# The last expert's gate logits summed ahead of its rows, and the wait for the result's last rows moved from GpSimd to VectorE

## The chip, the cores and the metric

One core of one Trainium2 chip runs the whole program. The metric is the device time of one execution in microseconds (us). Engine names as in the rows: PE is TensorE's matrix multiply, PEld its weight loads (the two overlap), DVE is VectorE, ACT is ScalarE, POOL is GpSimd, SP is the sync engine; a "q" behind a name (POOLq, SPq) is the engine's own queue of waits, branches and DMA issues.

## The reference, cut to what matters

Attention over 2 batches of 768 tokens comes first; its result, 1536 rows of 512 numbers, goes through two mixture-of-experts layers with 8 experts each. The first layer (`_moe_ref`) gives every expert exactly 192 tokens. The second one takes the first one's rows:

```
skip_score = x @ w_skip                 # rows with skip_score <= 0 pass unchanged
logits = x @ w_gate                     # 1536 x 8
e_idx  = argmax(logits); gate = softmax(logits)[e_idx]
out[i] = x[i] + gate * (relu(x[i] @ w1[e_idx]) @ w2[e_idx])
```

So nothing of the second layer can be placed before the first layer's rows have been multiplied with `w_gate` (8 columns) and `w_skip` (1 column). The kernel keeps the nine columns together.

## The kernel before, in words

`middle` is the first expert layer. Its work is a list of steps written out by `middle_plan`, and every engine walks the same list in that order and takes from it what is its own. For an expert k the steps are `xt` (transpose the gathered tokens), `h` (first matmuls, line 1006), `y` (second matmuls, line 1020, into transposed rows yT of 4 blocks d = 0 to 3, copied to SBUF by ACT at line 1093 two blocks at a time) and `rw` (line 1035). An `rw` step multiplies 96 rows of yT, two blocks of them, with `pw2`, 137 columns wide: 128 are an identity and turn the rows round, 9 are the gate columns. There are four `rw` steps per expert (two halves i of 96 rows, two pairs a of blocks). ACT copies from each first the partial logits into `lg4` (line 1100) and then the rows into `x1` (line 1101). For expert 7 nothing is left to fill the time, so its `rw` steps stand alone at the end of the list. All float32 matmuls appear as two records each in the trace: 8 matmuls of line 1035 are "x16".

`regroup` places rows for the second layer, in three batches; the third is the two row blocks of expert 7 (`place`, NI - 2, 2). DVE (`vector`) sums the four partial logits (line 1350), takes the best expert (lines 720 to 724), makes the one-hot O2 (line 1357), waits until PE has counted (`tensor`: four small bf16 matmuls, lines 1433 to 1439), computes places (lines 1362 to 1366) and a selection matrix `sel` (line 1370), and then the records (up to line 1384), which POOL scatters to DRAM (line 1455, two DMAs). `totals` (line 1446) is one bf16 matmul with 8 columns, which DVE's `table` waits for: the table says which further tiles run and is read by the engines late in the second layer.

`experts2` is the second layer. Its tile 0 is mixed: most rows come early by a gather (line 1546), transposed by `first_rows` (line 1552) into a PSUM bank, and expert 7's rows are added to the same bank by `last_rows` (line 1561) with `sel`. ACT copies the bank out (line 1692), then `hidden` (line 1650) and `rows` (line 1664) follow for every tile. Tiles from 1 on are gathered by POOL (line 1578) once SP has loaded their records (line 1615); `transposes` (line 1637) runs on PE between the two parts of `rows`. DVE adds (line 1709) into `ob`, POOL scatters `ob` to the output (line 1586). `tiles` is the helper that unrolls these steps for an engine, with a branch for the tiles that may not exist; its argument `last` is called after everything else of the tile, and it is `landed` for POOL: a wait until the scatter's data have landed. `K["warm"](bank, n)` issues n bf16 matmuls of 512 columns whose result nobody reads. They stand after `first_rows` (5) and at the head of `last_rows` (6). Before `last_rows`, PE waits for `sel` and for the last `x1` copy.

At the program's end (the block that ends at line 1723 in the trace) every engine runs a DRAIN, then all meet at a semaphore.

Of the kernel before, what the change touches and what calls it, by code (L numbers as in the profile page):

```python
# [10 lines left out]
ALU = mybir.AluOpType  # L11
ACT = mybir.ActivationFunctionType
AX = mybir.AxisListType
# [3 lines left out]
N, DM, E, F = B * S, H * D, 8, 1024  # L17
# [11 lines left out]
KD, KF = DM // P, F // P  # L29
# [575 lines left out]
HT = CAP // 2  # L605
# [19 lines left out]
def middle_plan():  # L625
# [67 lines left out]
    for k in range(ROUNDS - 1, E):  # L693
# [6 lines left out]
        steps += todo  # L700
    steps += [("rw", E - 1, i, a) for i in range(2) for a in range(2)] + [("place", NI - 2, 2)]
    return steps
# [24 lines left out]
def middle(nc, io, sb, sem, K, link):  # L727
# [73 lines left out]
    s_w1, s_w2 = K["s_w1"], K["s_w2"]  # L801
    K["s_lg"] = sem("logits_copied")
    K.update(s_x1=s_x1, s_x1l=s_x1l, s_f=s_f, s_e=s_e, s_tok=s_tok, use=use)
# [96 lines left out]
    def tensor(pe, place):  # L900
        for st in steps:
# [109 lines left out]
            elif st[0] == "y":  # L1011
# [11 lines left out]
                if part and d % 2:  # L1023
                    ins.then_inc(s_f, 1)
            elif st[0] == "rw":

                _, k, i, a = st
                ps = enter(pe, use[st])
                if i == 0 and a == 0:
                    pe.wait_ge(s_e, emptied(("y", k, KD // 2 - 1)))  # L1030
                    if k == 0:
                        pe.wait_ge(K["s_const2"], K["n_const2"])
                for c in range(2):
                    d = 2 * a + c
                    ins = nc.tensor.matmul(ps[0:HT, c * 137:c * 137 + 137], yT[:, k % 2, d, i * HT:(i + 1) * HT],  # L1035
                                           K["pw2"][:, d, :], start=True, stop=True)
                ins.then_inc(s_f, 1)
            elif st[0] == "place":
                place(pe, *st[1:])


    def scalar(act, place):
        for st in steps:
# [51 lines left out]
            elif st[0] == "rw":  # L1095
                _, k, i, a = st
                n = use[st]
                act.wait_ge(s_f, n + 1)
                v = psW[n % NWB][0:HT, 0:274].rearrange("p (c t) -> p c t", c=2)
                nc.scalar.copy(lg4[:, 2 * k + i, 2 * a:2 * a + 2, :], v[:, :, 128:137]).then_inc(K["s_lg"], 1)  # L1100
                nc.scalar.copy(x1[:, 2 * k + i, 256 * a:256 * a + 256].rearrange("p (c t) -> p c t", c=2),
                               v[:, :, 0:128]).then_inc(s_e, 1)
            elif st[0] == "place":
                place(act, *st[1:])
# [190 lines left out]
def regroup(nc, io, sb, sem, K, link):  # L1295
# [46 lines left out]
    def vector(dve, i0, n):  # L1342
# [3 lines left out]
        if b == 0:  # L1346
            nc.vector.memset(cum[:, :], 0.0)
            link(dve, nc.vector.memset(cumb[:, :], 0.0))
        dve.wait_ge(K["s_lg"], 2 * (i0 + n))
        link(dve, nc.vector.tensor_reduce(lg[:, 0:n, :], lg4[:, i2, :, :].rearrange("p i k n -> p i n k"), AX.X, ALU.add))  # L1350
        l8 = lg[:, 0:n, 0:E]
# [71 lines left out]
    def tensor(pe, i0, n):  # L1423
        if i0 + n == NI:
            K["first_rows"](pe)
            K["warm"](K["psA"][1][:, 0, :], 5)
        pe.wait_ge(s_o2, batches[i0, n] + 1)
# [10 lines left out]
        for k in range(1, n):  # L1438
            ins = nc.tensor.matmul(psP[0:HT, k * E:n * E], K["onesb"][0:HT, 0:HT], Of[:, 0:(n - k) * E], start=False,
                                   stop=k == n - 1, skip_group_check=True)  # L1440
        ins.then_inc(s_pp, 1)

    def totals(pe):
# [24 lines left out]
def experts2(nc, io, sb, sem, K):  # L1468
# [86 lines left out]
    def last_rows(pe):  # L1555
        K["warm"](K["psA"][1][:, 0, :], 6)
        pe.wait_ge(K["s_sel"], 1)
# [9 lines left out]
    def pool(gp):  # L1567
# [21 lines left out]

        def landed(t):  # L1590
            gp.wait_ge(s_st[t % 2], 16 * (t // 2 + 1))

        tiles(gp, gather, store, landed, ahead=2)

# [32 lines left out]
    def tensor(pe):  # L1627
        def transposes(t):
            if t == 0:
                last_rows(pe)  # L1630
                K["totals"](pe)
                return
# [49 lines left out]
        for t in range(E - 1):  # L1682
            hidden(t)
            rows(t, 0, 6)
            transposes(t + 1)
            rows(t, 6, KF)
# [15 lines left out]
    def vector(dve):  # L1702
# [9 lines left out]

        tiles(dve, nothing, add)

# [232 lines left out]
```

## Time and profile before

| | |
|---|---|
| time, median of 3 runs | 669.04 us (668.77 to 669.31) |
| the profiled execution's own time | 669.03 us |
| its span, first to last instruction | 667.2 us |
| PE busy | 637.5 us, 96% |
| PEld busy | 500.7 us, 75% |
| DVE, ACT, POOL busy | 366.5, 293.6, 155.8 us |
| mean granted TensorE clock | 0.994 of full |
| chain that ended last | PE 85%, issue 4%, DVE 4%, ACT 2% |

The profiled execution lies 1.8 us above its span and agrees with the median. PE is busy in nearly all of the span, so a change counts where PE waits: at the join of the layers (about 517 to 526 us), and after PE's last matmul (656.4 us), where the span goes on for 10.8 us. A timeline row gives start, length, engine, line, what is done, and in brackets how long the engine had been idle and what released it.

### The profile page before, as it was taken

The page shows a single profiled execution, that of the slowest core. Times are in us where ns is not written, and L with a number is a line of the kernel's source. Part 1 is how long each engine was busy: PE and PEld are TensorE (multiplying, and loading weights), DVE is VectorE, ACT ScalarE, POOL GpSimd, SP SyncE. Part 2 cuts the span into 40 slices and gives each one's busy share as a digit, 9 for nine tenths or more (in the row PEclk, how much of TensorE's full clock was granted, in tenths as well). Part 3 has the DMA queues.
Part 4 walks back from the last instruction along what each step waited for, and adds up shares of the span by engine and source line. Part 5 has one row for each costly group of instructions (what it writes and reads, how often), then busy time and mean ns, then how long its engine had stood idle before and what let it go on. Part 6 is the DMA issues. An engine that isn't in the chain of part 4 may idle for free.

```text
span 667.2 us, 11738 instructions
## 1 busy us (share of the span) xinstructions
PE 637.5 (96%) x4544; PEld 500.7 (75%) x4544; DVE 366.5 (55%) x1114; ACT 293.6 (44%) x551; POOL 155.8 (23%) x151
## 2 busy tenths in 40 slices
PE   6899999999999999989999999999999999999993
PEld 3667777777777665468898988989999766777771
DVE  5876777676776677787787868585301400000000
ACT  4767676767677667143543525251321211111110
POOL 5440313031320943201010101101161232223100
PEclk9999999999999999999999999999999999999997
DMA  8975646454562300554362717354996599999910
GB/s 205 227 170 127 145 99 160 121 119 119 121 197 63 77 21 1 201 171 151 128 201 77 273 57 246 133 169 151 342 331 225 171 312 357 362 335 325 330 69 8
DMA packets 73758, 118.40 MB, mean 177 GB/s; under 512 B 33400, under 2 KB 36600, under 8 KB 73426
## 3 DMA queue, kind: packets, MB, share of 16 engines
q1 hardware_dynamic: 69298, 108.65, 52.6%
q0 software_dynamic: 4080, 8.93, 4.0%
q8 instruction: 38, 0.62, 0.4%
q14 instruction: 22, 0.18, 0.1%
q10 hardware_dynamic: 320, 0.01, 0.0%
HBM read 88.07 MB, written 12.36 MB: 151 GB/s over the span
## 4 chain that ended last, share of the span: by engine, by line
PE 85%; issue 4%; DVE 4%; ACT 2%; POOL 1%; DMA 1%; SPq 0%; DVEq 0%; POOLq 0%
PE psB L1006 13%; PE psB L1020 12%; PE psB L1650 10%; PE psB L1664 9%; PE psB L311 8%; PE psB L296 8%; PE psA L281 6%; PE psA L283 4%; PE psB L1035 2%; PE psA L940 2%; PE psB L326 2%; PE psB L258 2%; PE psB L250 1%; DVE mx L431 1%; PE psB L1793 1%
## 5 line engine op out<-in xcount | busy, mean ns | idle before, releaser
L431 DVE TENSOR_REDUCE mx<-psA 128x1 f32<-128x768 f32 x96 | 91.8, 957 | 48.7 <-PE psA L283 47.1
L549 ACT ACTIVATE prob<-psA,ebi,esc 128x768 f32<-128x768 f32 x96 | 95.8, 998 | 30.6 <-DVE ebi L377 30.6
L1006 PE MATMUL psB<-xgT,w 128*128 128x192 f32 x512 | 92.8, 332 | 3.0 <-ACT xgT L1080 3.0
L1006 PEld LDWEIGHTS psB<-xgT,w 128*128 128x128 f32 x512 | 82.4, 190 | 9.0 <-ACT xgT L1080 3.7
L1020 PE MATMUL psB<-hT,w 128*128 128x192 f32 x512 | 88.6, 329 | 0.0
L1020 PEld LDWEIGHTS psB<-hT,w 128*128 128x128 f32 x512 | 82.7, 190 | 0.3
L296 PE MATMUL psB<-cst,prob 128*128 128x128 f32 x576 | 78.8, 273 | 0.4
L281 PE MATMUL psA<-kH,qT 128*128 128x384 f32 x192 | 74.1, 386 | 1.9 <-DMA kB<-kbits 1.1
L542 ACT COPY pT<-psB 128x512 f32<-128x512 f32 x96 | 56.5, 588 | 41.1 <-PE psB L296 39.9
L1709 DVE SCALAR_TENSOR_TENSOR ob<-psB,recs,xg 128x512 f32<-128x512 f32 x9 | 6.8, 751 | 121.1 <-PE psB L1664 121.1
L296 PEld LDWEIGHTS psB<-cst,prob 128*128 128x128 f32 x576 | 67.6, 140 | 6.4 <-DVE pT L444 2.3
L1650 PEld LDWEIGHTS psB<-xgT,w 128*128 128x128 f32 x576 | 65.6, 192 | 4.7 <-issue 4.7
L311 PE MATMUL psB<-pT,v_in 128*64 128x384 f32 x360 | 68.0, 499 | 0.0
L1650 PE MATMUL psB<-xgT,w 128*128 128x128 f32 x576 | 65.8, 275 | 0.8 <-ACT xgT L1692 0.8
L283 PE MATMUL psA<-kB,qB 128*128 128x384 f32 x192 | 64.9, 338 | 0.0
L1664 PE MATMUL psB<-w,hT 128*128 128x512 f32 x144 | 64.6, 592 | 0.0
L281 PEld LDWEIGHTS psA<-kH,qT 128*128 128x128 f32 x192 | 36.1, 188 | 30.7 <-issue 28.1
L1250 POOL DMA_INDIRECT xg<-x_scratch,sidx x16 | 15.3, 958 | 182.5 <-DVE sidx L1142 180.0
L1664 PEld LDWEIGHTS psB<-w,hT 128*128 128x128 f32 x144 | 26.0, 190 | 26.3 <-issue 26.3
L571 POOL CAST hi<-raw 128x768 fp32r<-128x768 f32 x16 | 14.1, 890 | 127.2 <-ACT raw L522 111.0
L1086 ACT ACTIVATE hT<-psB 128x384 f32<-128x384 f32 x32 | 15.7, 491 | 60.4 <-PE psB L1006 60.2
L1697 ACT ACTIVATE hT<-psB 128x512 f32<-128x512 f32 x18 | 10.8, 597 | 68.4 <-PE psB L1650 68.4
(259 smaller groups left out, 903.5 us busy)
## 6 DMA issues: line engine op xcount, KB each, us to landing
w<-in_moe_w SPq DMA_DIRECT2D x34, 2048.0 KB, 9.6
kH<-hi SPq DMA_DIRECT2D x30, 192.0 KB, 3.5
q_in<-in_q SPq DMA_DIRECT2D x16, 192.0 KB, 3.5
k_in<-in_k SPq DMA_DIRECT2D x16, 192.0 KB, 4.0
v_in<-in_v SPq DMA_DIRECT2D x8, 384.0 KB, 3.4
x_scratch<-x_of_batch SPq DMA_DIRECT2D x2, 1536.0 KB, 6.9
x_scratch<-x SPq DMA_DIRECT2D x8, 384.0 KB, 10.6
qT<-hi SPq DMA_DIRECT2D x15, 192.0 KB, 3.5
```

The lines of the kernel that those rows point to most:

```text
L281: nc.tensor.matmul(psS[u % 2][:, half, 0:HALF], qT[:, i, hh, qs], kH[:, i, hh, ks], start=True, stop=False)
L283: ins = nc.tensor.matmul(psS[u % 2][:, half, 0:HALF], qB[:, i, hh, qs], kB[:, i, hh, ks], start=False, stop=True)
L296: ins = nc.tensor.transpose(psT[part][:, at * P:(at + 1) * P], prob[:, u % 2, c // GU, c % GU * P:(c % GU + 1) * P], cst[:, C_ID:C_ID + P])
L311: ins = nc.tensor.matmul(psV[64 * hh:64 * hh + 64, 0:HALF], v_in[:, i, hh, c, :], pT[:, (2 * G + hh) % 4, c, :], start=c == 0, stop=c == N ...
L431: nc.vector.tensor_reduce(mx[:, u:u + 1], psS[u % 2][:, :, 0:HALF], AX.XY, ALU.max).then_inc(s_dv, 1)
L542: nc.scalar.copy(pT[:, (2 * G + hh) % 4, TD:NC_, c * P:(c + 1) * P], psT[1][:, 0:(NC_ - TD) * P].rearrange("p (c q) -> p c q", c=NC_ - TD) ...
L549: ins = nc.scalar.activation(prob[:, u % 2, :, :], psS[u % 2][:, :, 0:HALF], ACT.Exp, bias=ebi[:, u:u + 1], scale=esc[:, u:u + 1], accum_o ...
L1006: ins = nc.tensor.matmul(ps[:, (f % 2) * CAP:(f % 2 + 1) * CAP], w1[:, k % 2, d, f * P:(f + 1) * P], xgT[:, k % 2, d, :], start=d == 0, st ...
L1020: ins = nc.tensor.matmul(ps[:, (d % 2) * CAP:(d % 2 + 1) * CAP], w2[:, k % 2, f, d * P:(d + 1) * P], hT[:, k % 2, f, :], start=f == 0, sto ...
L1086: nc.scalar.activation(hT[:, k % 2, f - 1:f + 1, :], psW[n % NWB][:, 0:2 * CAP].rearrange("p (c t) -> p c t", c=2), ACT.Relu).then_inc(s_e, 1)
L1650: ins = nc.tensor.matmul(psH[q][:, f * P:(f + 1) * P], w1[:, k2 % 2, k, (4 * q + f) * P:(4 * q + f + 1) * P], xT[:, t % 2, k, :], start=k ...
L1664: ins = nc.tensor.matmul(psY[t % 2][:, :], hh[:, t % 2, f, :], w2[:, k2 % 2, f, :], start=f == 0, stop=f == KF - 1)
```

## The change

In the plan, a step `logits` stands before expert 7's `rw` steps. It sums expert 7's gate and skip logits in PSUM, 4 blocks by 2 halves, 8 float32 matmuls with 9 moving columns; blocks 0 and 1 only need the first yT copy. DVE waits for that (semaphore `s_ll`) and takes the sum from PSUM with one copy in place of the reduction; ACT no longer copies the partial logits of expert 7. `first_rows` moves behind the counting matmuls; both `warm` calls (11 matmuls) go; `totals` moves from behind `last_rows` to behind `hidden(0)`. In `experts2`, `landed` moves from POOL to DVE.

```diff
-    steps += [("rw", E - 1, i, a) for i in range(2) for a in range(2)] + [("place", NI - 2, 2)]
+    steps += [("logits", )] + [("rw", E - 1, i, a) for i in range(2) for a in range(2)] + [("place", NI - 2, 2)]
...
+    K["psLog"] = psRow[1][0:HT, 0:2 * NW]
...
+            elif st[0] == "logits":
+                k = E - 1
+                for d in range(KD):
+                    if d % 2 == 0:
+                        pe.wait_ge(s_e, emptied(("y", k, d // 2)))
+                    for i in range(2):
+                        ins = nc.tensor.matmul(K["psLog"][:, i * NW:(i + 1) * NW], yT[:, k % 2, d, i * HT:(i + 1) * HT],
+                                               K["pw2"][:, d, 128:128 + NW], start=d == 0 and i == 0,
+                                               stop=d == KD - 1, skip_group_check=True)
+                ins.then_inc(K["s_ll"], 1)
...
-                nc.scalar.copy(lg4[:, 2 * k + i, 2 * a:2 * a + 2, :], v[:, :, 128:137]).then_inc(K["s_lg"], 1)
+                if k < E - 1:
+                    nc.scalar.copy(lg4[:, 2 * k + i, 2 * a:2 * a + 2, :], v[:, :, 128:137]).then_inc(K["s_lg"], 1)
...
-        dve.wait_ge(K["s_lg"], 2 * (i0 + n))
-        link(dve, nc.vector.tensor_reduce(lg[:, 0:n, :], lg4[:, i2, :, :].rearrange("p i k n -> p i n k"), AX.X, ALU.add))
+        if i0 + n < NI:
...
+        else:
+            dve.wait_ge(K["s_ll"], 1)
+            link(dve, nc.vector.tensor_copy(lg[:, 0:n, :], K["psLog"].rearrange("p (i n) -> p i n", n=NW)))
...
     def tensor(pe, i0, n):
-        if i0 + n == NI:
-            K["first_rows"](pe)
-            K["warm"](K["psA"][1][:, 0, :], 5)
         pe.wait_ge(s_o2, batches[i0, n] + 1)
...
         ins.then_inc(s_pp, 1)
+        if i0 + n == NI:
+            K["first_rows"](pe)
...
     def last_rows(pe):
-        K["warm"](K["psA"][1][:, 0, :], 6)
         pe.wait_ge(K["s_sel"], 1)
...
-        def landed(t):
-            gp.wait_ge(s_st[t % 2], 16 * (t // 2 + 1))
-
-        tiles(gp, gather, store, landed, ahead=2)
+        tiles(gp, gather, store, ahead=2)
...
                 last_rows(pe)
-                K["totals"](pe)
                 return
...
             hidden(t)
+            if t == 0:
+                K["totals"](pe)
             rows(t, 0, 6)
...
-        tiles(dve, nothing, add)
+        def landed(t):
+
+            dve.wait_ge(s_st[t % 2], 16 * (t // 2 + 1))
+
+        tiles(dve, nothing, add, landed)
```

## Rows read from the trace of the kernel before

**Rows 1.** The page, part 4: chain that ended last, by engine.
```profile
PE 85%; issue 4%; DVE 4%; ACT 2%; POOL 1%; DMA 1%; SPq 0%; DVEq 0%; POOLq 0%
```

**Rows 2.** Timeline of the join: start, length, engine, line, [idle before <-releaser].
```profile
506.35 10.56 PE L1020 MATMUL psB<-hT,w 128*128 128x192 f32 x64
...
517.54 1.89 PEld L1035 LDWEIGHTS psB<-pw,yT 128*96 128x96 f32 x16 [0.93 <-ACT yT L1093]
517.57 2.09 PE L1035 MATMUL psB<-pw,yT 128*96 128x137 f32 x16 [0.66 <-ACT yT L1093]
...
519.61 0.97 PEld L1552 LDWEIGHTS psA<-cst,xg 128*128 128x128 f32 x8 [0.18 <-DMA xg<-x_scratch,recs]
...
519.77 0.37 ACT L1101 COPY x<-psB 96x256 f32<-96x256 f32 x1
...
520.28 0.17 DVE L720 TENSOR_REDUCE best<-lg 96x2 f32<-96x16 f32 x1
...
521.80 0.12 PEld L1433 LDWEIGHTS psA<-O,strictb 96*96 96x96 bf16 x1 [0.45 <-DVE O L1357]
...
522.25 0.17 DVE L1362 TENSOR_TENSOR tmp<-psA,cst 96x16 f32<-96x16 f32 x1 [0.43 <-PE psA L1439]
...
523.59 1.86 PEld L1561 LDWEIGHTS psA<-sel,x 96*128 96x128 f32 x16 [0.62 <-DVE sel L1370]
...
525.67 0.59 ACT L1692 COPY xgT<-psA 128x512 f32<-128x512 f32 x1 [3.96 <-PE psA L1561]
...
526.40 7.38 PE L1650 MATMUL psB<-xgT,w 128*128 128x128 f32 x64 [0.76 <-ACT xgT L1692]
```

**Rows 3.** Instruction groups, 517.4 to 526.4 us: count | busy us, mean ns.
```profile
L1793 PE MATMUL psA<-onesb 128*128 128x512 bf16 x11 | 2.7, 378 | 0.0
```

**Rows 4.** The timeline at 492 us: a run of float32 weight loads.
```profile
492.38 0.80 PEld L992 LDWEIGHTS psB<-cst,xg 96*128 96x128 f32 x8
```

**Rows 5.** Timeline, 520 to 539 us: what feeds the second tile.
```profile
520.22 0.33 SPq L1264 DMA_DIRECT2D x_scratch<-x  x1
...
526.52 0.92 POOL L1455 DMA_INDIRECT records<-rec,posi  x1 [0.30 <-issue]
...
529.07 2.25 SPq L1615 DMA_DIRECT2D recs<-records  x5
...
533.20 0.96 POOL L1578 DMA_INDIRECT xg<-x_scratch,recs  x1 [0.30 <-issue]
...
533.82 0.38 SPq L1596 DMA_DIRECT2D w<-in_moe_w  x1
...
538.84 0.42 PEld L1637 LDWEIGHTS psA<-cst,xg 128*128 128x128 f32 x4 [0.72 <-DMA xg<-x_scratch,recs]
```

**Rows 6.** DMA issues, 517-532 and 476-495 us: last number is landing.
```profile
x_scratch<-x SPq DMA_DIRECT2D x1, 384.0 KB, 8.4
...
records<-rec,posi POOLq DMA_INDIRECT x2, 2.8
...
records<-rec,posi POOLq DMA_INDIRECT x10, 7.4
```

**Rows 7.** Busy time by stretch, with PEclk, DMA share, GB/s last.
```profile
526.00:527.00 1.00, 0.59 (x5) 0.63 (x6) 0.90 (x4) 0.26 (x1) 0.69 (x2) 1.00 0.36 130
...
659.00:660.00 1.00, 0.00 (x0) 0.00 (x0) 0.00 (x0) 0.00 (x0) 0.00 (x0) 0.67 0.24 84
```

**Rows 8.** Lines L1723 and L1510: count: duration ns min/median/max, first and last start.
```profile
L1723 DVEq DRAIN  x1: 582/582/582, 656.7 to 656.7; - x1
...
L1723 POOLq DRAIN  x1: 5547/5547/5547, 661.5 to 661.5; - x1
...
L1510 POOLq COMPARE_BRANCH  x1: 38/38/38, 660.6 to 660.6; - x1
```

**Rows 9.** The timeline at the end: the last two operations.
```profile
656.43 0.75 DVE L1709 SCALAR_TENSOR_TENSOR ob<-psB,recs,xg 128x512 f32<-128x512 f32 x1 [13.26 <-PE psB L1664]
657.98 0.98 POOL L1586 DMA_INDIRECT out<-ob,recs  x1 [13.00 <-DVE ob L1709]
```

More of the change, by code:

```diff
@@ L801, in middle @@
     s_w1, s_w2 = K["s_w1"], K["s_w2"]
-    K["s_lg"] = sem("logits_copied")
+    K["s_lg"], K["s_ll"] = sem("logits_copied"), sem("last_logits")
+    K["psLog"] = psRow[1][0:HT, 0:2 * NW]
     K.update(s_x1=s_x1, s_x1l=s_x1l, s_f=s_f, s_e=s_e, s_tok=s_tok, use=use)
@@ L1348, in vector @@
             link(dve, nc.vector.memset(cumb[:, :], 0.0))
-        dve.wait_ge(K["s_lg"], 2 * (i0 + n))
-        link(dve, nc.vector.tensor_reduce(lg[:, 0:n, :], lg4[:, i2, :, :].rearrange("p i k n -> p i n k"), AX.X, ALU.add))
+        if i0 + n < NI:
+            dve.wait_ge(K["s_lg"], 2 * (i0 + n))
+            link(dve, nc.vector.tensor_reduce(lg[:, 0:n, :], lg4[:, i2, :, :].rearrange("p i k n -> p i n k"), AX.X,
+                                              ALU.add))
+        else:
+            dve.wait_ge(K["s_ll"], 1)
+            link(dve, nc.vector.tensor_copy(lg[:, 0:n, :], K["psLog"].rearrange("p (i n) -> p i n", n=NW)))
         l8 = lg[:, 0:n, 0:E]
```

## The prediction

> **What bounds the kernel now.** I read the chain that ended last first: 85% of it is PE and the rest is waits of a few tenths [rows 1]. So an edit pays only where PE stands still with nothing queued, or behind its last matmul. Then the timeline of the join. Expert 7's last `y` matmul ends at 506.35 + 10.56 = 516.91. ACT copies it, and PE's `rw` steps start at 517.57 (0.66 idle) and end at 519.66 [rows 2]. After that PE has `first_rows` (from 519.61) and 11 matmuls that only fill time [rows 2, 3]; what the next layer really waits for is a chain that crosses engines: `rw` full, ACT copies the last logits, DVE reduces them and begins its choice at 520.28, PE counts at 521.80, DVE goes on at 522.25, `sel` lets `last_rows` start at 523.59, ACT copies at 525.67, `hidden` starts at 526.40 [rows 2]. From there on PE is fed without a break but for one short wait (0.72 on the weight-load side at 538.84, for the second tile's gather [rows 5]). So every tenth by which that chain starts earlier is a tenth of the time, until another input is late. Last the tail: DVE's last add ends at 656.43 + 0.75 = 657.18, POOL issues the last scatter at 657.98 to 658.96 [rows 9], its queue wakes on the landing at 660.6, begins its DRAIN at 661.5 and needs 5.547 us for it; all else is long done [rows 8]. That ends the span at 667.2.
>
> **The join, step by step.** The new `logits` step has 8 matmuls, 16 records, with yT as weights (128x96, as in `rw`) and only 9 moving columns, so weight loads set its pace. No row has such a matmul. The dearest near row is `rw` itself with 137 columns: 1.89 / 16 = 0.118 us a record [rows 2]. A run with 96 moving columns goes at 0.80 / 8 = 0.10 [rows 4]. The lower end is that it costs nothing, since half of it fits into the 0.66 us that PE idles anyway. I take 0.10, the nearest in columns and in what limits it: from 516.91, 8 records to 517.71 (the gap is gone), 8 more to 518.51; the yT copy is in by 517.54, so the second half doesn't wait.
>
> The `rw` steps then end at 518.51 + 2.09 = 520.60, 0.95 later than before. DVE starts its copy when the last logits matmul is through, about 0.3 after its load (518.8), and this costs about what a 96x16 read of PSUM costs, 0.17 [rows 2], so the choice begins at about 519.0 and not at 520.28: 1.28 earlier. Counting could then start at 521.80 - 1.28 = 520.52, and PE's queue is free at 520.60. The two meet; I book 521.80 - 520.60 = 1.2. At 0.118 a record PE is the later one: 516.91 + 1.89 + 2.09 = 520.89, which leaves 0.9. At a price of zero PE is free at 519.66 and the gain is at most 2.1. Both ends go into the range.
>
> The Trainium skill (TensorE: Matmul & The Clock Gate, section LDWEIGHTS) says a weight load takes its columns divided by 1.2, in ns, whatever the rows, so 80 ns for 96 columns. By that the step would take 16 x 0.08 = 1.28 us and the join would gain 1.5 instead of 1.2. No row here shows a load at that pace, the nearest goes at 0.10, so the sum doesn't use it.
>
> Behind the count nothing is longer than it was. `first_rows` (a run that begins at 519.61 and takes about 1.1 with the matmuls' tail) now stands between count and `last_rows`: it runs from about 520.8 to 521.9, inside the time in which DVE makes `sel` (before: 521.80 to 523.59, 1.79 [rows 2]; now 520.6 to 522.4). That cover is 0.5 longer than it needs. Its gather had landed at 519.6 [rows 2], over a microsecond before it is now wanted; if the cover were gone it would cost up to 1.1. The two `warm` runs, 2.7 busy us in all [rows 3], stood wholly in waits, so taking them out gives and costs nothing in itself. ACT's last row copy (519.77 before [rows 2]) comes at about 520.7 and ends at 521.1, ahead of `last_rows` at 522.4. ACT has four small copies less, which nobody waited for any more. `totals` stood in a wait of PE; now it stands between two full runs: one more bf16 load, as the 0.12 of line 1433 [rows 2], so minus 0.1. DVE's table starts some 7 us later than now and nobody reads it before the second half of the layer, and DVE's next add comes at about 540; so nothing.
>
> What is late next is the second tile. The chain of records moves with DVE: second scatter at 526.52 - 1.2 = 525.3, records loaded from 529.07 - 1.2, gather from 533.20 - 1.2 [rows 5]. The weights of line 1596 (533.82) move as well, as they wait for PE, so the two compete as before [rows 5]. But two things don't move: the DMA engines are full until 526 to 527 [rows 7], so the scatters are now in that crowd, and the last `x1` store goes from 520.22 to about 521.1 and lands 8.4 later [rows 5, 6], at 529.5 at most (before: 528.6). POOL waits for it ahead of its gathers; it would look at it from 529.8. That holds by 0.3. A few tenths of delay to the gather, 0 to 0.5, are likely and partly already in the 0.72; I take 0.1. The join is then worth 1.2 - 0.1 - 0.1 = 1.0, from 0.4 to 1.9.
>
> **The tail.** POOL now has no wait for landings. Its engine is free at 658.96 [rows 9]. Whether its queue gets to the DRAIN at once or after its branches isn't shown; they and the waits took 661.5 - 660.6 = 0.9 before [rows 8]. DVE's DRAIN starts at 656.7, inside its last add that ends at 657.18, so a queue does run ahead of its engine [rows 8, 9]. Whatever DRAIN does for 5.547 us, POOL had been idle for 2.5 us when it began [rows 8, 9]: it didn't wait for POOL's own instruction. If the length is its own, it now ends between 658.96 + 5.55 = 664.5 and 0.9 later, where it was 667.0: a gain of 1.6 to 2.5, and I take 2.2. DVE takes the wait over: behind it there is only its DRAIN. Landing at 660.6 plus 0.9 for the same waits plus 0.58 is 662.1, over 2 us ahead of POOL, so that costs nothing; if POOL's DRAIN were short, DVE would end the span.
>
> A sentence on what could be inside: the Trainium skill (GPSIMD Engine Reference, section Instruction dispatch) says that the first call of a freshly loaded routine pays about 6 us with no instruction to be seen; that would make the length fixed, and the sum the same. No row here shows that a load takes place.
>
> **Sum.** 669.03 (the profiled execution, 667.2 span and 1.8 around it; the median is 669.04) - 1.0 - 2.2 = 665.8.
>
> **The rivals.**
> (a) As above: 665.8, by itself 664.8 to 667.0. Chance 0.55.
> (b) The DRAIN only begins its 5.55 us when the last data have landed: 660.6 + 5.55 = 666.15 and not 667.0, 0.9 gained, 667.1 in all. For it: all that is outstanding then is that scatter. Against it: before, nothing was outstanding, and it was long even so. Chance 0.15.
> (c) The edit of the tail does nothing: the end of the DRAIN hangs on the last DMA instruction (8.0 us after its end now), not on when the DRAIN starts. Then only the join counts: 669.03 - 1.0 = 668.0. For it: 5.5 us on an idle engine look like waiting for something. Chance 0.20.
> (d) Slower: the scatters of records, now issued at 524.1 and 525.3 into full DMA engines, land 7.4 us after issue, as in the crowd at 476 to 495 us, and not 2.8 [rows 6]. Records, gather and the second tile's transposes would be 4.6 later, and PE would stand at about 537.5 for that long: 669.03 - 1.0 + 4.6 - 2.2 = 670.4. It decides once the crowd lasts to 529 us or so. Against it: at 526 to 527 the engines are busy for only 0.36 [rows 7], and the bytes are the same. Chance 0.05.
> (e) Slower or no gain: without the fill matmuls the clock falls at the join. After the last matmul at 656.4 the granted clock is at its full level (2.4 GHz) still for over two microseconds and falls to the half in 659 to 660 [rows 7]. PE's longest rests at the join would be about 0.5 to 0.8, as now, and at 526 to 527, after such a rest, the clock was full [rows 2, 7]. If it fell, `hidden(0)`'s 7.38 us would take up to as much again, 670 and more. The rule of the Trainium skill (TensorE: Matmul & The Clock Gate, Part 1) that activity holds the clock up speaks against taking filler out; the rests are too short here for me to give it more than this. Chance 0.05.
>
> **How the numbers follow.** The forecast is (a), 665.8. The range must leave out no more than 2 in 10: from 664.7 (the join at 1.8, the tail at 2.5) to 668.3 (case (c) with a weaker join); (d), (e) and the edges lie outside. What a measurement of this kernel can tell from no change is 0.2%, 1.3 us, so below 667.7 is faster: (a), nearly all of (b) and a third of (c), 0.76. Same: the rest of (c) and some of (b) and (e), 0.16. Slower: 0.08.
>
> **What the profile after should show.** Line 1350's reduction is gone for this batch and DVE's choice begins near 519.0. The logits run lasts about 1.6 with no idle time ahead of it; if it lasts 1.9, the join gives 0.9. `last_rows` starts near 522.4, `hidden` near 525.2. At line 1637's first run, the wait for the gather is at most 1.2; if it is several us, (d). Granted clock 1.00 from 518 to 530; if not, (e). POOL's DRAIN begins at 659 to 660 and lasts 5.5: (a). If it lasts 7: (b). If it ends 8 us after the scatter's end whatever its start: (c). The forecast is wrong by most if the DRAIN's length isn't its own.

## The result and the profile after

| | before | changed |
|---|---|---|
| median of 5 runs | 669.04 us | 666.74 us |
| lowest to highest | 668.77 to 669.91 | 664.87 to 670.08 |
| ratio | | 0.9963, 95% interval 0.9945 to 0.9982 |
| profiled execution, span and own time | 667.2, 669.03 | 668.3, 670.08 |

The changed kernel is 2.3 us faster in the median. Its five executions spread over 5 us and those of the kernel before over 1, and the profiled execution is its slowest. Some executions of several kernels ran far slower (745, 925, 2251 us); medians and ratios here leave them out.

With more executions the difference in spread is smaller: 24 of the kernel before lie within 3.5 us (668.2 to 671.6, standard deviation 1.0), 12 of the changed one within 5.8 (e10_after below, 1.7). Part of the spread comes from ahead of the join. There, in this profile, the granted clock was at half (1.2 GHz) for 3.4 us from 288.3 on, and the first 16 matmuls of line 1009 took 4.52 us (first row); in e3_hold (described below), with the clock full, they took 2.84 (second row):

```profile
287.56 4.52 PE L1009 MATMUL psB<-xgT,w 128*128 128x192 f32 x16 [0.33 <-ACT xgT L1093]
```

```profile
288.16 2.84 PE L1009 MATMUL psB<-xgT,w 128*128 128x192 f32 x16 [0.33 <-ACT xgT L1093]
```

So the profile is read against the end of the last `y` matmul: 507.41 + 10.56 = 517.97, before 516.91 [rows 2], 1.06 later. But for the first weight loads of the logits nothing of the change stands ahead of that mark, and it lies between 516.9 and 519.4 from one kernel's profile to the next on the chips of the first result and of the first and last experiments.

The timeline of the changed kernel at the join and through its second tile:

```profile
507.41 10.56 PE L1023 MATMUL psB<-hT,w 128*128 128x192 f32 x64
...
517.65 1.65 PEld L1034 LDWEIGHTS psA<-pw,yT 128*96 128x96 f32 x16
...
518.01 0.48 ACT L1106 COPY yT<-psB 128x384 f32<-128x384 f32 x1 [4.72 <-PE psB L1023]
...
519.24 2.10 PE L1048 MATMUL psB<-pw,yT 128*96 128x137 f32 x16
...
519.70 0.17 DVE L721 TENSOR_REDUCE best<-lg 96x2 f32<-96x16 f32 x1
...
521.22 0.12 PEld L1449 LDWEIGHTS psA<-O,strictb 96*96 96x96 bf16 x1
...
521.42 1.14 PE L1570 MATMUL psA<-cst,xg 128*128 128x128 f32 x8
...
523.00 2.05 PE L1578 MATMUL psA<-sel,x 96*128 96x128 f32 x16 [0.44 <-DVE sel L1389]
...
525.82 7.38 PE L1663 MATMUL psB<-xgT,w 128*128 128x128 f32 x64 [0.77 <-ACT xgT L1707]
525.93 0.92 POOL L1473 DMA_INDIRECT records<-rec,posi  x1 [0.30 <-issue]
529.67 2.24 SPq L1629 DMA_DIRECT2D recs<-records  x5
...
533.23 0.38 SPq L1610 DMA_DIRECT2D w<-in_moe_w  x1
...
533.49 0.96 POOL L1595 DMA_INDIRECT xg<-x_scratch,recs  x1 [0.30 <-issue]
...
540.67 0.93 PE L1650 MATMUL psA<-cst,xg 128*128 128x128 f32 x4 [2.21 <-DMA xg<-x_scratch,recs]
...
541.39 3.35 PE L1677 MATMUL psB<-w,hT 128*128 128x512 f32 x4
```

The sum of logits (line 1034) begins ahead of the last `y` matmul's end. The rows' `rw` steps (line 1048) start 1.27 after it, DVE's choice (line 721) at +1.73 (519.70; before 520.28 - 516.91 = +3.37), the count (line 1449) at +3.25 (before +4.89), `last_rows` (line 1578) at +5.03 (before +6.68), `hidden` (line 1663) at 525.82 - 517.97 = +7.85, before +9.49 [rows 2]. So TensorE is 1.64 us ahead as it enters the second layer. Then it loses all of it and more: the second tile's transposes (line 1650) wait 2.21 us for their gather, and the matmuls behind them take 3.35 for 4 where four like them take 1.88 elsewhere. The stretches of the same execution (PE, PEld, DVE, ACT, POOL busy, then PEclk, DMA share, GB/s) show why:

```profile
539.00:540.60 1.60, 0.00 (x0) 0.00 (x0) 0.00 (x0) 0.00 (x0) 0.00 (x0) 1.00 1.03 422
540.60:542.00 1.40, 1.32 (x5) 1.06 (x6) 0.00 (x0) 0.36 (x1) 0.00 (x0) 0.61 0.77 313
542.00:544.00 2.00, 2.00 (x4) 0.72 (x3) 0.00 (x0) 0.22 (x1) 0.00 (x0) 0.50 0.00 0
544.00:545.00 1.00, 1.00 (x6) 0.71 (x5) 0.22 (x1) 0.00 (x0) 0.00 (x0) 0.83 0.00 0
545.00:546.00 1.00, 1.00 (x11) 1.00 (x10) 0.53 (x1) 0.00 (x0) 0.00 (x0) 1.00 0.07 20
```

TensorE stood still from about 538.5 to 540.7. A mean of 0.61 over the 1.4 us from 540.6 is full clock (2.4 GHz) for 0.3 and half (1.2 GHz) for the rest, so it fell at 540.9; by the 0.83 it came back at about 544.3. The DMA engines are full (share 1.03) while TensorE waits for the gather; in this execution the wait was followed by a second loss, through the clock.

The tail, the last two operations and the DRAINs (kind, count, duration ns, start):

```profile
659.96 0.75 DVE L1724 SCALAR_TENSOR_TENSOR ob<-psB,recs,xg 128x512 f32<-128x512 f32 x1 [13.26 <-PE psB L1677]
661.50 0.98 POOL L1603 DMA_INDIRECT out<-ob,recs  x1 [13.00 <-DVE ob L1724]
```

```profile
L1742 POOLq EVENT_SEMAPHORE  x2: 17/17/17, 668.1 to 668.2; - x2
...
L1742 POOLq DRAIN  x1: 6603/6603/6603, 661.4 to 661.4; - x1
...
L1742 DVEq DRAIN  x1: 17/17/17, 665.0 to 665.0; - x1
```

POOL's DRAIN starts at 661.4, ahead of the scatter it stands behind, and ends at 668.0, 5.56 after the scatter's end at 662.48. Before, it ended 8.05 after it (661.46 + 5.55 against 658.96 [rows 8, 9]). VectorE is through at 665.0, 3 us earlier. The tail gives 2.5 us.

The three parts add up to the profiled execution. VectorE's last add starts 659.96 - 517.97 = 141.99 after the mark, before 656.43 - 516.91 = 139.52: 669.03 + 1.06 (ahead of the join) + 2.47 (join to last add) - 2.49 (tail) = 670.07, measured 670.08.

### The profile page after: what moved, and what is told of

Its sections match the earlier page's. It is cut to its first block, busy times and chain, and to the rows that moved or that the text cites. A ratio compares the mean times of both kernels' runs of the same rounds, so it can differ in the third digit from the quotient of the medians.

```text
span 668.3 us, 11743 instructions
## 1 busy us (share of the span) xinstructions
PE 638.6 (96%) x4549; PEld 503.6 (75%) x4549; DVE 366.5 (55%) x1114; ACT 292.9 (44%) x547; POOL 155.1 (23%) x151
## 4 chain that ended last, share of the span: by engine, by line
PE 80%; DMA 5%; issue 4%; DVE 4%; SPq 3%; ACT 2%; POOL 2%; POOLq 0%; DVEq 0%
PE psB L1009 14%; PE psB L1023 12%; PE psB L1677 9%; PE psB L1663 9%; PE psB L311 8%; PE psB L296 7%; PE psA L281 5%; PE psA L283 4%; PE psB L1048 2%; PE psA L943 2%; PE psB L326 2%; DMA xg<-x_scratch,recs 1%; DMA kB<-kbits 1%; PE psB L1812 1%; PE psB L250 1%
## 5 line engine op out<-in xcount | busy, mean ns | idle before, releaser
L1009 PE MATMUL psB<-xgT,w 128*128 128x192 f32 x512 | 94.5, 336 | 3.0 <-ACT xgT L1093 3.0
L1009 PEld LDWEIGHTS psB<-xgT,w 128*128 128x128 f32 x512 | 84.1, 193 | 9.0 <-ACT xgT L1093 3.7
L1663 PEld LDWEIGHTS psB<-xgT,w 128*128 128x128 f32 x576 | 65.8, 192 | 5.1 <-issue 5.1
L1677 PE MATMUL psB<-w,hT 128*128 128x512 f32 x144 | 66.2, 604 | 0.0
```

The costliest lines, as they stand in the source:

```text
L1009: ins = nc.tensor.matmul(ps[:, (f % 2) * CAP:(f % 2 + 1) * CAP], w1[:, k % 2, d, f * P:(f + 1) * P], xgT[:, k % 2, d, :], start=d == 0, st ...
L1663: ins = nc.tensor.matmul(psH[q][:, f * P:(f + 1) * P], w1[:, k2 % 2, k, (4 * q + f) * P:(4 * q + f + 1) * P], xT[:, t % 2, k, :], start=k ...
L1677: ins = nc.tensor.matmul(psY[t % 2][:, :], hh[:, t % 2, f, :], w2[:, k2 % 2, f, :], start=f == 0, stop=f == KF - 1)
```

## The experiments

**The two edits apart.** e1_tail is the kernel before with this alone:

```diff
-        def landed(t):
-            gp.wait_ge(s_st[t % 2], 16 * (t // 2 + 1))
-        tiles(gp, gather, store, landed, ahead=2)
+        tiles(gp, gather, store, ahead=2)
...
-        tiles(dve, nothing, add)
+        def landed(t):
+            dve.wait_ge(s_st[t % 2], 16 * (t // 2 + 1))
+        tiles(dve, nothing, add, landed)
```

> The kernel before with one edit: VectorE and not GpSimd waits for the result's rows (the function landed). In the changed kernel GpSimd's DRAIN began at 661.4, inside the last scatter (661.50 to 662.48), and ended 5.56 us after the scatter's end; before it ended 8.05 us after it. Theory A (DRAIN costs its own 5.55 us as soon as the engine is free): 2.5 us faster than before, 666.5, with as little spread as before (about 1 us). Theory B (part of what the changed kernel won at the tail was something of that one execution): less than 1 us faster, DRAIN ends 8 us after the scatter.

Measured: 666.57 us median, the kernel before beside it 669.28; ratio 0.9960 (0.9945 to 0.9975), so 1.7 to 3.7 us faster. Its executions spread over 4.1 us (665.5 to 669.61), without any of the join's edits. The last scatter and the DRAIN:

```profile
658.18 0.98 POOL L1586 DMA_INDIRECT out<-ob,recs  x1 [13.00 <-DVE ob L1706]
```

```profile
L1724 POOLq DRAIN  x1: 6603/6603/6603, 658.1 to 658.1; - x1
```

The DRAIN ends 5.56 after the scatter, as in the changed kernel. The tail's edit is worth 2.5 us in both profiles, and the median agrees.

e2_join is the changed kernel with that edit taken back (the diff above the other way round).

> The changed kernel with GpSimd waiting for landings again, so only the join's edits are left. Theory A (the race: TensorE reaches the second tile's transposes 1.6 us earlier, the gather for them comes only 0.8 earlier and now starts behind the 2 MB weight load that TensorE's progress releases; by execution it lands in time or up to 3 us late, and after a long wait the clock falls as well): between 667.4 (in time) and 672.6, a spread of some 5 us, median about 669.2, no faster than before. Theory C (the spread comes from the head of the program, the half-clock stretch at 288 us, and the join's gain is whole): 1.6 us faster, 667.4, with a second cluster 1 us above.

Measured: 669.66 against 669.28, ratio 1.0002 (0.9986 to 1.0019). Ten of its runs lie between 667.3 and 671.5, one at 673.0. So the join's edits give nothing that the median can show, though they make `hidden` start 1.64 earlier in each profile of theirs. My second theory, that the spread comes from the half-clock stretch near 288 us and the join's gain is whole, holds only in its first half: the stretch is in this profile too (289.3 to 292.7), but a whole gain would have shown in the median. The profile has the mild form of the late gather, a wait of 0.51 us at line 1653:

```profile
530.38 2.25 SPq L1632 DMA_DIRECT2D recs<-records  x5
...
534.20 0.96 POOL L1595 DMA_INDIRECT xg<-x_scratch,recs  x1 [0.30 <-issue]
...
534.62 0.38 SPq L1613 DMA_DIRECT2D w<-in_moe_w  x1
...
540.36 0.66 PE L1653 MATMUL psA<-cst,xg 128*128 128x128 f32 x4 [0.51 <-DMA xg<-x_scratch,recs]
```

**The late gather.** In e3_hold SyncE waits for it before it issues the weights that compete with it:

```diff
                 sp.wait_ge(s_h, 2 * (t - 1))
+                if t == 2:
+                    sp.wait_ge(s_g[1], 16)
                 w1_load(sp, t, io["moe2_w1"][bass.ds(e, 1), :, :])
```

> The changed kernel; SyncE waits until the second tile's rows have been gathered before it issues the third tile's first weights (line 1610, t = 2). Theory A (the race with the weight load): the gather lands about 3 us earlier than in the changed kernel's profile (537.5 and not 540.6), TensorE's wait at line 1650 is under 0.3 us, no half-clock stretch at 541; 664.9, all executions within 1 us but for the head's stretch at 288 us (+1). Theory C (the gather is late because its records are late, not because of the weights): the wait stays over 1 us and the spread stays. The weights themselves are wanted 18 us later, so holding them for 3 us costs nothing in either.

Measured: 664.9 (663.96 to 666.07) against 669.28, ratio 0.9925 (0.9906 to 0.9945). The gather is issued at 532.18, the weights at 535.82, the transposes (line 1652) start at 537.19 with no wait, the clock is full there:

```profile
528.34 3.10 SPq L1629 DMA_DIRECT2D recs<-records  x5
...
532.18 0.96 POOL L1595 DMA_INDIRECT xg<-x_scratch,recs  x1 [0.30 <-issue]
...
535.82 0.38 SPq L1610 DMA_DIRECT2D w<-in_moe_w  x1
...
537.19 0.60 PE L1652 MATMUL psA<-cst,xg 128*128 128x128 f32 x4
```

That is 1.7 us below e1_tail and 1.8 below the changed kernel: with the gather in time the join's gain is whole. The transposes start 20.34 after the last `y` matmul's end (516.85); in the changed kernel's profile 540.67 - 517.97 = 22.70.

e4_swap goes at it from the other side. The second tile's records and gather go first and nothing waits:

```diff
         def gather(t):
+            t = 1 - t if t < 2 else t
             gp.wait_ge(s_rl[t], 16)
...
                 sp.wait_ge(K["s_rsl"], 16 * 2)
+            t = 1 - t if t < 2 else t
```

> The changed kernel; GpSimd gathers the second tile's rows before those that VectorE adds to the first tile, and SyncE loads the second tile's records first. Nothing waits for the weights. Theory A (the second tile's gather comes too late behind the weight load): it is issued 1.3 us earlier, at about the same distance ahead of the weights as in the kernel before, TensorE's wait at line 1650 is 0 to 0.5 us, PE ends 137.8 to 138.4 us after the last y matmul (changed kernel's profile: 141.95), median 664.9 to 665.5. Theory C (the wait is set by the records alone): the gather moves by 1.3 all the same, so this can't tell the two apart, but if the wait stays over 1 us in the profile neither holds.

This kernel, e6_drain, e7_tail_hold and e8_crowd ran on another chip, on which everything was some 9 us longer (the kernel before: 678.63), nearly all of it ahead of the join; only ratios compare. Measured: 0.9926 (0.9900 to 0.9952), as e3_hold; the gather is issued at 540.85, the weights at 541.68, and the transposes start at +20.35, no wait.

e7_tail_hold adds the hold of e3_hold to e1_tail.

> The kernel e1_tail (the kernel before with only the tail's edit) with the hold of e3_hold: the third tile's first weights wait for the second tile's gather. Theory A: in the kernel before the gather comes in time, so the hold brings 0 to 0.2 us: 666.6, PE ends 139.4 us after the last y matmul; the difference to e3_hold, 1.6 to 1.7 us, is then the join's gain when nothing takes it back. Rival: the hold itself is a gain of 1 us or more (weights that load in the gather's way also slow other things), 665.5 or less, and the join's edits are worth under 1 us even at their best.

Measured: 0.9951 (0.9932 to 0.9970); e1_tail had 0.9960. The difference, 0.6 us, is smaller than either interval, and the profiles show none: VectorE's last add starts 666.12 - 526.72 = 139.40 after the last `y` matmul, in e1_tail 656.64 - 517.23 = 139.41. So the hold alone brings nothing that shows. Beside it on the same chip e4_swap is at 0.9926, 0.0025 x 678.6 = 1.7 us better. The intervals overlap, but its profile has 137.89, 1.5 earlier, as have all six profiles with the join's edits and the gather in time (e3_hold, e4_swap, e6_drain, e8_crowd, e9_drain_early, e12_best: 137.9). That is the join with nothing taken back.

e10_after is the changed kernel again.

> The changed kernel once more, unchanged, beside the kernel before on the same chip, for another profile of the race. In the profiles so far the second tile's gather lands 7.1 us after its issue where the weights were issued 0.3 us ahead of it, 6.1 where they came 0.4 behind it, 5.6 at 0.6, 4.6 at 0.8 and 3.6 at 1.6 or held back. Theory A: this profile's gather lies on that line as well, and TensorE's wait follows from it; the executions spread over some 3 to 5 us, median 2.3 to 3 us below the kernel before, above e3_hold's 5. Rival (the first result was drawn down by single bad executions): median 4 us or more below the kernel before, as the kernels with the gather in time.

Measured: 667.07 against 669.0, ratio 0.9968 (0.9951 to 0.9984), 12 runs from 664.94 to 670.7. It is as in the first result, and the rival, that single bad executions had drawn the first result down, is out. The profile has a 3.26 us wait, on line 1650:

```profile
532.19 0.96 POOL L1595 DMA_INDIRECT xg<-x_scratch,recs  x1 [0.30 <-issue]
532.24 0.38 SPq L1610 DMA_DIRECT2D w<-in_moe_w  x1
...
540.73 0.66 PE L1650 MATMUL psA<-cst,xg 128*128 128x128 f32 x4 [3.26 <-DMA xg<-x_scratch,recs]
...
541.23 1.88 PE L1677 MATMUL psB<-w,hT 128*128 128x512 f32 x4
```

The weights were issued 0.05 us behind the gather, which landed 8.5 us after its issue. Here the clock stayed full, and the four matmuls took 1.88. The profiles side by side (gather and weights from the timelines; landing from the DMA view, where the trace has it; wait of TensorE's matmuls at the transposes):

| kernel | weights issued after the gather by | gather lands after | TensorE waits |
|---|---|---|---|
| changed | -0.26 | 7.1 | 2.21, and half clock |
| changed, again (e10_after) | 0.05 | 8.5 | 3.26 |
| e2_join | 0.42 | 6.1 | 0.51 |
| before | 0.62 | 5.6 | 0.1 (0.72 of the weight loads) |
| e11_before_drain | 0.66 | 5.8 | 0.2 |
| e1_tail | 0.81 | 4.6 | 0 |
| e4_swap | 0.83 | not in the trace | 0 |
| e5_warm | 1.61 | 3.6 | 0 |
| e9_drain_early, e12_best (held) | 3.4 | 3.3, 3.4 | 0 |
| e3_hold | 3.64 | 3.6 | 0 |

It isn't a line, as my expectation had it. With 0.8 us of lead or more the gather lands within 4.6 us, with less than 0.7 it takes 5.6 or more; among the late ones the order isn't strict, since the worst (8.5) had the weights just behind it and not ahead. And TensorE asks for the rows at +20.3 with the join's edits, at +21.9 without them, so the kernel before could bear 5.6 and the changed one can't. Each kernel has one profile, so how its other executions divide between the gather, the clock and the part ahead of the join isn't shown.

**What makes the gather lose its lead.** TensorE, and with it the weights, came 1.64 earlier; the gather only 0.77 (533.49 - 517.97 = +15.52, before 533.20 - 516.91 = +16.29) or 1.07 (e10_after, +15.22). The last scatter of records is a full 1.65 earlier (525.93: +7.96; before +9.61), but SyncE can load records only at +11.70, before +12.16: the scatter takes 3.74 to be seen and not 2.55 (in e10_after 3.43, in e2_join 3.06). In e8_crowd the 2 MB load that fills the DMA engines at that time comes later:

```diff
         sp.wait_ge(K["s_f"], K["use"][("y", E - 2 + t, KD // 2 - 1)] + 1)
-        w2_load(sp, t, io["moe2_w2"][t:t + 1])
+        if t == 0:
+            w2_load(sp, t, io["moe2_w2"][t:t + 1])
...
         def body(t):
+            if t == 1:
+                sp.wait_ge(s_g[1], 16)
+                w2_load(sp, t, io["moe2_w2"][t:t + 1])
```

> The changed kernel, but the second tile's second weights (2 MB, issued at 516.9 to 518.0 so far and filling the DMA engines until 526 to 527) are loaded only after the second tile's gather has landed. Theory F (that load is the crowd which holds up the scatters of the last records): the records land 2.5 us or less after the second scatter's start, as in the kernel before, and not 3.5 to 3.7; records are loaded by SyncE 1.0 us earlier against the last y matmul than in e3_hold (+10.5 and not +11.5), the gather as well; time 664.9 as e3_hold, since there TensorE doesn't wait any more. Rival (the landing is late for the scatter's own reasons): records load stays at +11.5.

```profile
534.00 0.92 POOL L1473 DMA_INDIRECT records<-rec,posi  x1 [0.30 <-issue]
536.80 1.77 SPq L1630 DMA_DIRECT2D recs<-records  x4
```

536.80 - 534.00 = 2.8, against 3.5 in e3_hold (528.34 against 524.82) and 3.74 in the changed kernel. Against the last `y` matmul (526.03) the records are loaded at +10.77 and not +11.49. In the nine profiles with the join's edits and that load in place the time is 3.06 to 3.91, so the load is most of the delay, 0.7 of it against e3_hold. Ratio 0.9925 (0.9900 to 0.9951), as e3_hold, since TensorE no longer waited there.

**The fill matmuls.** e5_warm puts them back where they stood:

```diff
             K["first_rows"](pe)
+            K["warm"](K["psA"][1][:, 0, :], 5)
...
     def last_rows(pe):
+        K["warm"](K["psA"][1][:, 0, :], 6)
```

> The changed kernel with its 11 fill matmuls put back, 5 behind first_rows and 6 ahead of last_rows. Theory A (they only stood in waits, and the late gather makes the slow executions): same median and same spread as the changed kernel, 665 to 670. Theory B (taking them out made the clock fall, and this is what costs): the spread goes, all executions near 664.9 to 665.5. A third possibility, that they now stand in the way since first_rows and they fill more than the wait for sel: 0.3 to 0.8 us slower than the changed kernel.

Measured: 666.9 (665.52 to 668.41), ratio 0.9956 (0.9937 to 0.9976). Of my three, the third possibility: the fill matmuls now stand in the way, and by more than I had put it. In the median it is no slower than the changed kernel, because that one loses as much to its late gather. The rows:

```profile
520.01 2.10 PE L1048 MATMUL psB<-pw,yT 128*96 128x137 f32 x16
...
525.55 1.95 PE L1580 MATMUL psA<-sel,x 96*128 96x128 f32 x16
```

`last_rows` (line 1580) starts 525.55 - 518.74 = +6.81 and not +5.03. Behind the count and `first_rows` the 11 matmuls run for 2.5 us, past the moment at which `sel` is ready, and take the join's whole gain back. The gather is in time for the same reason, so the kernel is e1_tail again in its times. It says nothing of the clock; there the profiles do: in none of e3_hold, e4_swap, e8_crowd, without fill matmuls, does the granted clock fall at the join (it is 1.00 from the last `y` matmul to the second tile).

**What a DRAIN costs.** e6_drain is e3_hold with one more, in the middle of the second layer:

```diff
                                   ).then_inc(s_st[t % 2], 16)
+            if t == 5:
+                gp.drain()
```

> The kernel e3_hold with one more DRAIN on GpSimd behind the sixth tile's scatter, in the middle of the second layer, where GpSimd has 8 us and more of rest. Theory D (a DRAIN behind a scatter takes 5.55 us each time): the extra one takes 5.5 to 6.6 us, hidden, the last one as well, time as e3_hold, 664.9. Theory E (only the first one of the program is dear, a routine that has to be brought in): the extra one 5.5 to 6.6 us, the last one under 1.5 us (its overlap with the scatter), 659.5 to 660.5, and VectorE's wait for the landing ends the span instead.

```profile
L1607 POOLq DRAIN  x1: 9182/9182/9182, 624.8 to 624.8; - x1
```

```profile
L1746 POOLq DRAIN  x1: 2911/2911/2911, 667.8 to 667.8; - x1
...
L1746 DVEq DRAIN  x1: 17/17/17, 671.4 to 671.4; - x1
```

The extra one takes 9.2 us in a rest of GpSimd, where both theories had 5.5 to 6.6; the last one takes 2.9 and ends 1.9 behind the scatter's end, which fits neither. VectorE's starts at 671.4 and ends the span. Ratio 0.9890 (0.9865 to 0.9914). Whether the first DRAIN is dear, or each one in proportion, was for e9_drain_early (the extra DRAIN behind the first layer's gathers):

> The kernel e3_hold with the extra DRAIN on GpSimd not in the second layer but behind the last of the 16 gathers of the first one, ahead of 51 of the 67 DMAs that GpSimd issues. In e6_drain (7 DMAs between the two DRAINs) the last DRAIN ended 1.9 us after the last scatter's issue and not 5.6. Theory E (a routine is brought in once, and was lost after the DRAIN at the program's start): the last one is as short as in e6_drain, 1.9 us after the scatter, VectorE ends the span, 2.5 to 3 us faster than e3_hold. Theory G (a DRAIN works off what the DMAs since the DRAIN before have left behind): 51 of 67 are left, the last one ends 4 us or more after the scatter, 0.5 to 1.5 us faster than e3_hold.

```profile
L1268 POOLq DRAIN  x1: 10122/10122/10122, 466.7 to 466.7; - x1
```

```profile
L1745 POOLq DRAIN  x1: 5281/5281/5281, 656.6 to 656.6; - x1
```

The last one starts at 656.57, just ahead of the scatter (656.63 to 657.61), and ends 4.24 behind it. Ratio 0.9926 (0.9904 to 0.9947), 663.9 us, 1.0 below e3_hold's median, where the profiles differ by 1.3 in the tail. e11_before_drain puts the extra DRAIN into the kernel before, and nothing else:

> The kernel before with only the extra DRAIN of e6_drain behind the sixth tile's scatter; GpSimd still waits for the landings at the end, as before. Theory E and G both: the last DRAIN, begun after the landing, loses 3.7 us or more of its 5.55. What the remaining 1.9 us of e6_drain was: if it was the wait for the landing (that DRAIN ended 0.2 us after VectorE saw it), the last DRAIN here takes under 0.5 us and the kernel is 5.1 to 5.5 us faster than before; if it was work of its own, it takes 1.9 us and the kernel is 3.7 us faster. Either is more than the change's own edit of the tail brought (2.5).

```profile
L1590 POOLq DRAIN  x1: 9681/9681/9681, 615.4 to 615.4; - x1
```

```profile
L1725 POOLq DRAIN  x1: 473/473/473, 662.0 to 662.0; - x1
```

The last DRAIN takes 0.473 us on an idle engine; 664.43 against 669.0, ratio 0.9926 (0.9906 to 0.9945). GpSimd issues 67 DMAs in all, and by the timelines 51 stand behind the extra DRAIN of e9_drain_early and 5 behind that of e6_drain and e11_before_drain (not 7 or 6, as the expectations have it). Per DMA since the DRAIN before that is 5.547 / 67 = 0.083, 4.24 / 51 = 0.083, 0.473 / 5 = 0.095; or 0.082 for each and 0.07 once, which fits all three. The simplest reading is that a DRAIN works off something that the DMAs leave; theory E's routine is out. The start of the program says the same: the DRAIN there, ahead of every DMA and so the first of all, takes 0.17 us.

```profile
L1938 POOLq DRAIN  x1: 169/169/169, 0.3 to 0.3; - x1
```

Whether it goes by DMAs or by their rows isn't shown: a DMA has 96 or 128 rows by the kernel's text, 7040, 5504 and 608 in the three cases, which makes 0.79, 0.77 and 0.78 ns a row.

In e6_drain 5 x 0.083 doesn't explain 1.9; there the DRAIN began as the scatter did. In e12_best below, the same kernel on another chip, the trace has that scatter's landing: 2.6 after its start, at 659.3, and the DRAIN ends at 659.55. So a DRAIN that has little to work off ends with the landing of what is in flight. The two DRAINs behind 62 DMAs are longer than that: in e11_before_drain 62 x 0.083 = 5.1 us from the scatter's end (616.64) would be over at 621.8, the scatter lands at 622.5 (6.9 after issue), and the DRAIN ends at 625.09, 2.6 behind the landing; in e12_best it is also 2.6. The one in e9_drain_early, behind only 16 DMAs, takes 10.1 us and ends 0.7 behind its last gather's landing (468.18 + 8.0 = 476.2). That they wait for the landing fits; what fills the 2.6 us behind it stays open.

**The best of it.** e12_best is e6_drain on a chip like the first.

> The kernel e6_drain once more (the changed kernel, the hold of e3_hold, and the extra DRAIN behind the sixth tile's scatter), with its times on another chip: on the first one everything ran some 9 us longer, the kernel before too. By the sum: 1.6 us from the join, 5.0 to 5.5 us from the tail (8.3 us from the last scatter's end to the end of the span, now 2.8), 0.1 from the second tile's wait: 6.9 to 7.2 us faster than the kernel before, 661.9 to 662.2. Theory G (0.083 us of DRAIN for each DMA since the DRAIN before: 5.55 for 67, 4.24 for 51, 0.47 for 6): the last DRAIN is short of work and ends with the landing, 0.2 us after it, and VectorE's wait ends the span.

```profile
656.70 0.98 POOL L1603 DMA_INDIRECT out<-ob,recs  x1 [13.00 <-DVE ob L1728]
```

```profile
L1746 POOLq DRAIN  x1: 2918/2918/2918, 656.6 to 656.6; - x1
```

Measured: 662.21 (661.07 to 662.27) against 669.11, ratio 0.9887 (0.9858 to 0.9915): 6.9 us faster than the kernel before and 4.5 to 4.9 below the changed one. VectorE's last add starts 655.15 - 517.27 = 137.9 after the last `y` matmul, before 656.43 - 516.91 = 139.5; the span ends at 660.5, 2.8 behind the scatter, before 8.3.

## Why the prediction was right, and where it wasn't

The time (666.74 for 665.8) lies in the range and its sign is right. The sum that led to it had the mechanism of two terms right and booked both a little low (0.44 at the join, 0.3 at the tail), and missed what happens in the third, which takes back about 2. So that the time came within 1 us of the forecast is partly luck: the errors cancelled in part.

- The join up to `hidden`: forecast 1.2, measured 1.64 in each profile of it (525.82 - 517.97 = 7.85, before 9.49). The step that was mis-sized is where the logits start. Their pace was as taken: 16 records in 1.65, 0.103 each. (The row it was taken from loads weights of 128 columns [rows 4], not 96 as here; the two paces are alike all the same.) But I let the first begin at the last `y` matmul's end, and weight loads run ahead of it: 517.65 against 517.97. So `rw` started at +1.27, and not at +1.6, DVE's choice at +1.73 and not +2.1, and the count wasn't held by TensorE but by DVE.
- The estimate of 80 ns for a load of 96 columns, from the Trainium skill's columns over 1.2 (TensorE: Matmul & The Clock Gate, section LDWEIGHTS), isn't what this step shows, 0.103 us a record; the measurement decides. That its sum of 1.5 came nearer to 1.64 than mine is by the early start.
- `first_rows` behind the count, ACT's copies, the selection: nothing was late there; `last_rows` waited for `sel`, as forecast. `totals` cost 0.1 (`hidden` to the second tile's transposes takes 12.48 in e3_hold and 12.37 in e1_tail).
- The second tile: forecast 0.1, measured 2.21 and 3.26 of wait in the two profiles of the changed kernel, once with 1.5 to 1.7 more through the half clock, and 0.51 in e2_join's. This is the step that failed. I had all its rows: the gather landing as TensorE wanted it, the weights issued 0.62 behind the gather, the scatters moving into full DMA engines [rows 5, 7]. I wrote that gather and weights move alike and compete as before. They don't: the weights hang on TensorE and came 1.64 earlier, the gather hangs on a landing in DRAM and came 0.8 to 1.1 earlier, and with a lead of 0.6 the difference takes the lead away. The delay of the records themselves was 0.5 to 1.2 in the three profiles (3.06, 3.43 and 3.74 against 2.55), where I had given 0 to 0.5.
- Rival (d) had the right place, but the wrong transfer: not the records for 4.6 us, but the gather behind the weights. Rival (e): the clock did fall in one profile, but behind a wait of 2.2 us for data in the second tile, and not at the join, where the fill matmuls had stood. The rule of the Trainium skill that I had cited (TensorE: Matmul & The Clock Gate, Part 1, activity holds the clock up) agrees with the fall after that rest; in e10_after the clock stayed full over a longer one, 3.26, so a rest of that size needn't bring it down.
- The tail: forecast 2.2 (1.6 to 2.5), measured 2.5 in each profile. It is the upper end, since the queue had run ahead: the DRAIN began as the scatter did (661.44 and 661.50), much as DVE's begins inside its add. Rivals (b) and (c) are out for this kernel. But the reason that I named beside (a), a routine brought in once (the Trainium skill, GPSIMD Engine Reference, section Instruction dispatch), is out as well: the first DRAIN of the program takes 0.17 us, and two extra DRAINs left the last one a length that goes with the DMAs between. (c) had a grain of truth, that on an idle engine it worked off the DMAs of before.
- The sum by what the runs showed: 1.64 + 2.49 = 4.1 with the gather in time (664.9, e3_hold's median, and the changed kernel's best runs, 664.9), less 0.5 to 3.3 of wait in the three profiles, less 1.7 in one of them for the clock. The medians say that some 2 us of it are lost in a typical execution.

## What to carry to other kernels

When a chain of small steps is shortened, look for a transfer whose start hangs on the faster side and another that hangs on a slower side, and compare their lead before and after: here 0.6 us of lead was all that a 256 KB gather had ahead of a 2 MB load, and one semaphore wait on the load gave the whole gain back. A kernel whose spread grows may have such a race in it; read the profile of a bad execution before tuning further, and read it from a mark close to the change. And look behind the last useful instruction: 8.3 us of this span came after the last scatter's end, waiting and an engine's closing work. Moving the wait alone took 2.5 of them, one idle-time DRAIN alone 5.1 (3.2 left in e11_before_drain), both together 5.5.

## What the runs showed of the hardware that I had not expected

- GpSimd's last DRAIN takes 0.08 us for each DMA issued since the DRAIN before (5.547 for 67, 4.24 for 51, 0.473 for 5; or 0.78 ns for each row), even when it begins 0.9 us after the last landing on an idle engine, and it can be paid ahead of time in a rest, where it took 9.2 to 10.1 us.
- A gather of 128 rows of 2 KB landed 3.3 to 3.6 us after its issue when the 2 MB load was held back or came 1.6 us later, and 5.6 to 8.5 when it was issued within 0.7 us of it.
- The granted clock fell to half 0.2 us after TensorE had resumed from a rest of 2.2 us, not in the rest, so the work behind the wait paid (3.35 for 1.88); after a rest of 3.26 in another execution it did not fall.
- The same small scatter of 96 records, issued while a 2 MB load still filled the DMA engines and not as it ended, was seen 3.1 to 3.9 us after issue and not 2.6.
